# Slot 0 of a mixture-of-experts stage loaded under a count-dependent wait, and zero rows written in eight later pieces

## The chip, the cores and the metric

One core of a Trainium2 chip runs the whole kernel. The metric is the device time of one execution in microseconds; lower is better. The engines are PE (TensorE, matrix products), DVE (VectorE), ACT (ScalarE), POOL (GpSimd) and SP (SyncE, which here only issues DMAs). Each runs its own stream of instructions in program order, and semaphores hold the streams together.

## What is computed

Two attention steps, then a mixture of experts, then a dense block, all in 32-bit floats. Cut from the reference:

```python
# attention: batch 8, heads 8, seq 576, head_dim 64, 32 packs
p_packed = sm_attn(p, k, v)                  # softmax(scale * p k^T) v
out = sm_attn(q, p_packed, p_packed)
# x: 4608 tokens (batch, seq) of 512
logits = x @ w_gate                          # 8 experts
expert_idx = np.argmax(logits, axis=1)
gate_w = probs[np.arange(N), expert_idx]
for e in range(8):
    xe = x[expert_idx == e]
    h = np.maximum(xe @ w1[e], 0.0)          # 512 -> 1024
    out[mask] = gate_w[mask, None] * (h @ w2[e])   # 1024 -> 512
# dense block on the result
r = np.maximum(x @ w_in, 0.0)                # 512 -> 2048
y = (s * (r * r) + b) @ w_out                # 2048 -> 512
```

## The kernel before

**Attention stage.** 16 units of one batch and four heads each; a unit is one iteration of every engine's loop (`for it in range(UNITS ...)`), and a batch is two units. SP loads k, q and v of unit u+2 into double buffers as PE lets go of them, and in every second unit one 512 KB chunk of expert 0's weights. In an iteration PE turns k and q, makes the scores, mixes values and packs; ACT takes the exponentials and the copies out of PSUM; DVE takes maxima and sums, writes the finished rows of x into `x_rows`, and every second iteration works out each token's expert (`experts`) and its rank in that expert's list (`positions`), with PE's `ranks(b)` between them. `base` (`counts_so_far`) holds the count of tokens of each expert up to the batch last ranked.

**Rows by expert.** `rows_dram` has one region of 4608 + 128 rows for each expert. POOL's `scatter(b, j)` sends 96 rows of x, gate and token number, by an indirect DMA, to their places there; a batch has six, and counts 96 on `x_sent[b % 4]`. So that a slot of 128 rows that is not full reads zeros, the first 128 rows of every region are zeroed first: ACT issues one DMA for all eight regions before its first iteration, and POOL waits for it (`zeroed`) before the first scatter.

**Expert stage.** The lists are cut into slots of 128 tokens, an expert's slots one after the other, and an expert without tokens gets one slot. DVE works out small tables after the last ranks (`step(...)`, `tables`): for each slot the row to load (`x_at`), the row to write (`y_at`), the count of weight chunks it needs (`w_need`) and the weight buffer (`w_off`). For each slot s:

- ACT loads x (`load(s)`) into the one buffer `xin`; PE turns it (`slot_in`); ACT copies it out as the high part (`x_hi`), DVE subtracts to get the low part (`x_lo`).
- PE makes h = x w1 in 24 products (`slot_up`), ACT the relu, PE turns h (`slot_turn`), ACT and DVE split it (`h_hi`, `h_lo`), PE makes y = h w2 in 24 products (`slot_down`), ACT scales by the gate and writes y (`y_out_`).

PE's loop runs `slot_up(s)`, `slot_in(s+1)`, `slot_down(s-1)`, `slot_turn(s)`.

**Weights.** An expert has eight chunks (four of w1, four of w2), numbered on through all experts; n is the running number, `EARLY` is 8. SP may fetch chunk n when `conv` (chunks converted) is at n-1, into `raw[n % 2]`. A conversion makes a high part and a low part and then counts `conv`. Chunks 0 to 7 (expert 0) are converted in the attention stage; chunks 8 and 9 by ACT (`round_high`) and DVE (`round_low`), since their place in the second weight buffer is `x_rows`, which is free only when the scatters have landed; chunks 10 and up by POOL (`split`), which waits for all scatters and for `conv` 10 first. POOL may convert expert e's chunks when the expert before the last has made its last product:

```python
def release(o):
    done = pool.value_load(starts[0:1, bass.ds(o - 1, 1)], min_val=1, max_val=SLOTS)
    pool.wait_ge(y_full, done)
```

`release(2)` stands ahead of expert 2's chunks and waits for the last slot of expert 0, `release(3)` for that of expert 1.

**Dense stage.** Groups of 512 tokens on PE, with no part in the change.

What sets the order around the change is the order of the calls in each engine's block: ACT's `load(0)` waits for `tables` and for all of `x_sent`; behind it stand `round_high(8)`, `round_high(9)`, `x_hi(0)`. DVE ends `positions(7)`, makes the tables, then `round_low(8)`, `round_low(9)`, `x_lo(0)`, `x_lo(1)`, `h_lo(0)`.

## Time and profile before

| | |
|---|---|
| median of 3 runs | 1540.14 us (1539.99 to 1545.33) |
| the profiled execution | 1553.64 us, span 1551.9 us |
| PE busy | 1458.8 us, 94% of the span |
| DVE, ACT, POOL busy | 31%, 31%, 27% |
| chain that ended last | PE 90%, DVE 3%, issue 3%, DMA 1%, POOL 1% |
| DMA | 122.93 MB, mean 79 GB/s |

The span is the profiled execution from its first to its last instruction; the time beside it also holds what lies around the span. All times of the trace are counted from the span's start. In the span cut into 40 slices, PE's busy share and the granted clock (in tenths) are:

```profile
PE   6887369999999999998999999999999999999996
...
PEclk9899679999999999999999999999999999999998
```

The first five slices are the attention stage and the boundary behind it, the next thirteen the experts, the rest the dense stage. A slice is 38.8 us.

### The profile page before, as it was taken

Reading aid. Unit: us, or ns where it says so; the run is one execution under the profiler, and the core shown is the slowest. Engines: PE = TensorE matmul, PEld = TensorE weight load, DVE = VectorE, ACT = ScalarE, POOL = GpSimd, SP = SyncE. Lnnn points to the kernel's source line nnn. Section 1 sums busy time; section 2 is a strip of 40 time slices with the busy share of each in tenths; the row PEclk is TensorE's granted clock in tenths of the full one; section 3 lists DMA queues with packets and bytes.
Section 4 is the critical chain, followed back from the end, with each engine's and each line's share of the span. In section 5 each row is a group of like instructions: output and inputs, shape, how many; then the busy total and the mean of one; then the engine's idle time right before and its main releaser. Section 6 shows DMA issues by size and latency. Waiting matters only on the chain.

```text
span 1551.9 us, 24717 instructions
## 1 busy us (share of the span) xinstructions
PE 1458.8 (94%) x8664; PEld 1174.5 (76%) x8665; DVE 474.2 (31%) x808; ACT 480.3 (31%) x973; POOL 415.6 (27%) x278
## 2 busy tenths in 40 slices
PE   6887369999999999998999999999999999999996
PEld 5655258888888888886888888888888888888885
DVE  3777621111111111113523232322323232332322
ACT  5666123333333333332222222222222222222221
POOL 0244678448266557104501010100101010010100
PEclk9899679999999999999999999999999999999998
DMA  9688345234243343212101010100101000000000
GB/s 309 220 264 250 120 147 159 87 108 133 70 141 108 109 122 115 81 48 90 61 14 42 7 41 14 38 10 14 41 8 41 14 34 14 14 27 0 27 1 27
DMA packets 52860, 122.93 MB, mean 79 GB/s; under 512 B 6609, under 2 KB 12753, under 8 KB 52817
## 3 DMA queue, kind: packets, MB, share of 16 engines
q1 hardware_dynamic: 33728, 79.21, 16.8%
q10 hardware_dynamic: 13136, 24.19, 5.1%
q0 software_dynamic: 5952, 18.92, 3.4%
q8 instruction: 31, 0.51, 0.1%
q14 instruction: 13, 0.10, 0.0%
HBM read 90.78 MB, written 31.52 MB: 79 GB/s over the span
## 4 chain that ended last, share of the span: by engine, by line
PE 90%; DVE 3%; issue 3%; DMA 1%; POOL 1%; ACT 1%; another core or an unknown queue 0%; SPq 0%; ACTq 0%; DVEq 0%; POOLq 0%
PE psum L674 18%; PE psum L676 18%; PE psum L675 18%; PE psum L750 8%; PE psum L748 8%; PE psum L749 8%; PE psum L718 2%; PE psum L507 1%; PE psum L683 1%; PE psum L736 1%; PE psum L568 1%; PE psum L547 1%; POOL x_by_expert L418 1%; PE psum L609 1%; PE psum L622 1%
## 5 line engine op out<-in xcount | busy, mean ns | idle before, releaser
L1241 DVE SCALAR_TENSOR_TENSOR s_r_r<-r_relu,s_col 128x512 f32<-128x512 f32 x144 | 116.1, 806 | 450.4 <-ACT r_relu L972 450.4
L482 POOL DMA_INDIRECT out_dram<-out_sb,out_row_of_y x36 | 36.0, 1001 | 747.2 <-ACT out_sb L982 739.0
L674 PE MATMUL psum<-weights_split,gT_hi 128*128 128x512 f32 x576 | 230.8, 401 | 2.3 <-DVE gT_lo L1243 2.2
L972 ACT ACTIVATE r_relu<-psum 128x512 f32<-128x512 f32 x144 | 86.1, 598 | 471.7 <-PE psum L750 456.9
L675 PE MATMUL psum<-weights_split,gT_hi 128*128 128x512 f32 x576 | 227.7, 395 | 0.0
L676 PE MATMUL psum<-weights_split,gT_lo 128*128 128x512 f32 x576 | 227.6, 395 | 0.0
L750 PE MATMUL psum<-yT_hi,weights_split 128*128 128x512 f32 x576 | 227.2, 394 | 0.0
L748 PE MATMUL psum<-yT_hi,weights_split 128*128 128x512 f32 x576 | 226.1, 393 | 0.1
L749 PE MATMUL psum<-yT_lo,weights_split 128*128 128x512 f32 x576 | 225.8, 392 | 0.0
L396 POOL TENSOR_TENSOR weights_split<-weights_raw,one 128x1024 fp32r<-128x1024 f32 x70 | 135.5, 1936 | 253.9 <-PE psum L676 242.7
L398 POOL TENSOR_TENSOR weights_split<-weights_raw,weights_split 128x1024 fp32r<-128x1024 f32 x70 | 170.0, 2428 | 5.5
L1243 DVE SCALAR_TENSOR_TENSOR gT_lo<-s_r_r,b_col,gT_hi 128x512 fp32r<-128x512 f32 x144 | 114.4, 794 | 114.1 <-ACT gT_hi L975 113.3
L975 ACT ACTIVATE gT_hi<-s_r_r,b_col 128x512 fp32r<-128x512 f32 x144 | 104.3, 724 | 126.9 <-DVE s_r_r L1241 121.1
L674 PE MATMUL psum<-weights_split,hT_hi 128*128 x320 | 130.6, 408 | 4.7 <-issue 4.7
L674 PE MATMUL psum<-weights_split,xT_hi 128*128 x320 | 130.9, 409 | 2.8 <-DVE xT_lo L1217 2.8
L1223 DVE TENSOR_TENSOR hT_lo<-psum,hT_hi 128x512 fp32r<-128x512 f32 x80 | 51.5, 686 | 265.9 <-ACT hT_hi L908 265.9
L674 PEld LDWEIGHTS psum<-weights_split,gT_hi 128*128 128x128 f32 x576 | 108.3, 188 | 28.0 <-issue 2.4
L676 PEld LDWEIGHTS psum<-weights_split,gT_lo 128*128 128x128 f32 x576 | 108.2, 188 | 26.2
L749 PEld LDWEIGHTS psum<-yT_lo,weights_split 128*128 128x128 f32 x576 | 108.4, 188 | 25.8
L676 PE MATMUL psum<-weights_split,xT_lo 128*128 x320 | 127.6, 399 | 0.0
L675 PE MATMUL psum<-weights_split,xT_hi 128*128 x320 | 127.4, 398 | 0.0
L675 PE MATMUL psum<-weights_split,hT_hi 128*128 x320 | 127.2, 398 | 0.0
(151 smaller groups left out, 1832.4 us busy)
## 6 DMA issues: line engine op xcount, KB each, us to landing
weights_raw<-in_moe_w_dram SPq DMA_DIRECT2D x64, 512.0 KB
x_slot<-x_by_expert ACTq DMA_DIRECT2D x40, 257.0 KB, 2.8
y_sorted<-y_slot ACTq DMA_DIRECT2D x40, 256.5 KB, 3.3
k_sb<-in_k_dram SPq DMA_DIRECT2D x16, 576.0 KB, 6.5
q_sb<-in_q_dram SPq DMA_DIRECT2D x16, 576.0 KB, 7.7
v_sb<-in_v_dram SPq DMA_DIRECT2D x48, 192.0 KB
y_tile<-y_sorted SPq DMA_DIRECT2D x32, 256.5 KB, 2.7
weights_raw<-in_moe_w_in_dram SPq DMA_DIRECT2D x8, 512.0 KB
```

Of the source, the lines that this page charges most:

```text
L396: nc.gpsimd.tensor_tensor(hi, raw[c_ % 2][:], one[:].to_broadcast([P, CH]), ALU.mult).then_inc(hi_done, 1)
L398: nc.gpsimd.tensor_tensor(lo, raw[c_ % 2][:], hi, ALU.subtract).then_inc(conv, 1)
L674: nc.tensor.matmul(dst, lhs[0][:, col:col + P], rhs[0], start=first_, stop=False)
L675: nc.tensor.matmul(dst, lhs[0][:, col:col + P], rhs[1], start=False, stop=False)
L676: return nc.tensor.matmul(dst, lhs[1][:, col:col + P], rhs[0], start=False, stop=last_)
L748: nc.tensor.matmul(ps[:, HFB + f % 2, :], w[0], yT[0][:, k_, :], start=(k_ == 0), stop=False)
L749: nc.tensor.matmul(ps[:, HFB + f % 2, :], w[0], yT[1][:, k_, :], start=False, stop=False)
L750: last = nc.tensor.matmul(ps[:, HFB + f % 2, :], w[1], yT[0][:, k_, :], start=False, stop=(k_ == KD - 1))
L972: nc.scalar.activation(rel[:], ps[:, HFB + par, :], ACT.Relu).then_inc(rel_done, 1)
L975: nc.scalar.activation(gT[par][0][:], sq[par][:], ACT.Identity, bias=b_col[:]).then_inc(ghi_done, 1)
L1241: nc.vector.scalar_tensor_tensor(sq[par][:], rel[:], s_col[:], rel[:], ALU.mult, ALU.mult).then_inc(sq_done, 1)
L1243: nc.vector.scalar_tensor_tensor(gT[par][1][:], sq[par][:], b_col[:], gT[par][0][:], ALU.add, ALU.subtract).then_inc(glo_done, 1)
```

## The change

**Zero rows.** The one DMA of ACT becomes eight of 128 rows, issued in iterations 4 (three), 5 (three) and 6 (two), ahead of `out_pkt`. POOL waits for all eight, and sends batch 0's six scatters together after batch 2's logits.

**Slot 0's load.** It moves from ACT to SP, with a fixed address (the start of expert 0's region), behind chunk 8 and ahead of chunk 9. It no longer waits for the tables. What it waits for depends on `sent_need`, which DVE works out in iteration 15 from expert 0's count in batches 0 to 5: from 256 tokens up, only batches 0 to 5 must have landed (slots 0 and 1 are then complete), below that all eight. ACT's `load(1)` waits in the same way and for the tables.

**Order of slot 0's work.** PE takes slot 0 with fixed weights and without the tables right after `ranks(7)`: in, up, turn, then slot 1's in, slot 0's down; after it waits for the tables. ACT and DVE follow; the conversions of chunks 8 and 9 are placed anew.

```diff
@@ sync
             for n in (EARLY - 1, EARLY):
                 chunk(n % NCH, n, expert_chunk(n // NCH, n % NCH))
 
+            sp.wait_ge(need_done, 1)
+            sent = sp.value_load(sent_need[0:1, 0:1], min_val=BATCH_DMA, max_val=2 * BATCH_DMA)
+            for b in range(XBUFS):
+                sp.wait_ge(x_sent[b], 2 * BATCH_DMA if b < 2 else sent)
+            sp.wait_ge(t0_full, UNITS)
+            sp.wait_ge(t1_full, UNITS)
+            sp.dma_start(xin[:], rows_dram[0:P, :]).then_inc(xin_in, 16)
             for n in range(EARLY + 1, 2 * NCH):
                 chunk(n % NCH, n, expert_chunk(n // NCH, n % NCH))
@@ gpsimd
-                if b >= 2:
+                if b >= 3:
...
                 if b == 1:
-                    pool.wait_ge(zeroed, 16)
-                if b + 1 < B:
+                    round_low(2)
+                if b == 2:
+                    pool.wait_ge(zeroed, 16 * E)
+                    for j in range(J):
+                        scatter(0, j)
+                if 2 <= b and b + 1 < B:
                     scatter(b - 1, 0)
@@ tensor
             ranks(B - 1)
             pe.wait_ge(xa_done, UNITS)
-            pe.wait_ge(rank_read, B + 1)
-            pe.wait_ge(tables, 1)
...
             def slot_up(s):
-                ready = pe.value_load(w_need[0:1, bass.ds(s, 1)], min_val=KD, max_val=E * NCH)
-                buf = pe.value_load(w_off[0:1, bass.ds(s, 1)], min_val=0, max_val=WBUF)
+                ready, buf = KD, 0
+                if not isinstance(s, int) or s > 0:
+                    ready = pe.value_load(w_need[0:1, bass.ds(s, 1)], min_val=KD, max_val=E * NCH)
+                    buf = pe.value_load(w_off[0:1, bass.ds(s, 1)], min_val=0, max_val=WBUF)
...
-            before3 = pe.value_load(slots_m3[0:1, 0:1], min_val=N // P - 3, max_val=SLOTS - 3)
             slot_in(0)
             slot_up(0)
+            pe.wait_ge(rank_read, B + 1)
+            slot_turn(0)
             slot_in(1)
-            slot_turn(0)
-            with pe.Fori(1, before3 + 2) as s:
+            slot_down(0)
+            pe.wait_ge(tables, 1)
+            before3 = pe.value_load(slots_m3[0:1, 0:1], min_val=N // P - 3, max_val=SLOTS - 3)
+            slot_up(1)
+            slot_in(2)
+            slot_turn(1)
+            with pe.Fori(2, before3 + 2) as s:
@@ scalar
-            act.wait_ge(zeros_done, 1)
-            act.dma_start(rows_dram.rearrange("(e r) c -> r e c", e=E)[0:P],
-                          zeros[:].unsqueeze(1).to_broadcast([P, E, XW])).then_inc(zeroed, 16)
             for it in range(UNITS + 1):
...
+                if it == 4:
+                    act.wait_ge(zeros_done, 1)
+                if 4 <= it < 7:
+                    for e in range(3 * it - 12, min(3 * it - 9, E)):
+                        act.dma_start(rows_dram[e * REG:e * REG + P, :], zeros[:]).then_inc(zeroed, 16)
                 if it >= 1:
                     out_pkt(it - 1)
...
-            act.wait_ge(tables, 1)
-            before3 = act.value_load(slots_m3[0:1, 0:1], min_val=N // P - 3, max_val=SLOTS - 3)
-
-            for sent in x_sent:
-                act.wait_ge(sent, BATCH_DMA * B // XBUFS)
-            load(0)
+            act.wait_ge(x_sent[0], 2 * BATCH_DMA)
             round_high(EARLY)
             round_high(EARLY + 1)
             x_hi(0)
             keep_columns(0, 0)
+            act.wait_ge(need_done, 1)
+            sent = act.value_load(sent_need[0:1, 0:1], min_val=BATCH_DMA, max_val=2 * BATCH_DMA)
+            for b in range(XBUFS):
+                act.wait_ge(x_sent[b], 2 * BATCH_DMA if b < 2 else sent)
+            act.wait_ge(tables, 1)
+            before3 = act.value_load(slots_m3[0:1, 0:1], min_val=N // P - 3, max_val=SLOTS - 3)
             load(1)
             relu(0)
+            h_hi(0)
             x_hi(1)
             keep_columns(1, 1)
+            for sent in x_sent:
+                act.wait_ge(sent, 2 * BATCH_DMA)
             load(2)
-            h_hi(0)
@@ vector
+                if it == UNITS - 1:
+                    dve.wait_ge(rank_read, B - 1)
+                    nc.vector.tensor_scalar(few_first[:], base[0:1, 0:1], float(2 * P), float(BATCH_DMA), ALU.is_lt, ALU.mult).then_inc(few_done, 1)
...
+                if it == UNITS - 1:
+                    dve.wait_ge(few_done, 1)
+                    nc.vector.tensor_scalar_add(sent_need[:], few_first[:], float(BATCH_DMA)).then_inc(need_done, 1)
...
             positions(B - 1)
+            x_lo(0)
...
             nc.vector.tensor_tensor(y_at[:], x_f[:], x3[:, 2, :], ALU.subtract).then_inc(tables, 1)
+            dve.wait_ge(tables, 1)
+            before3 = dve.value_load(slots_m3[0:1, 0:1], min_val=N // P - 3, max_val=SLOTS - 3)
+            h_lo(0)
+            x_lo(1)
+            for sent in x_sent:
+                dve.wait_ge(sent, 2 * BATCH_DMA)
             round_low(EARLY)
             round_low(EARLY + 1)
-            dve.wait_ge(tables, 1)
-            before3 = dve.value_load(slots_m3[0:1, 0:1], min_val=N // P - 3, max_val=SLOTS - 3)
-            x_lo(0)
-            x_lo(1)
-            h_lo(0)
             with dve.Fori(1, before3 + 2) as s:
```

`slot_down` gets the same two lines as `slot_up`. The line numbers of the changed kernel differ from those of the kernel before.

**The order of instructions on DVE**, from the end of the slot tables to the slot loop, before (`slot_y_row` is the last of the tables, `weights_split` the conversions of chunks 8 and 9):

```order
L1204 CAST slot_row<-x_f 1x43 [waits rt]
L1205 TENSOR_TENSOR slot_y_row<-x_f,x 1x43
L1211 TENSOR_TENSOR weights_split<-weights_raw,weights_split 128x1024 [waits conv,hi_done] x2
L1226 TENSOR_LOAD slots_minus [waits tables]
L1226 ISA x2
L1217 TENSOR_TENSOR xT_lo<-psum,xT_hi 128x512 [waits xhi_done] x2
L1223 TENSOR_TENSOR hT_lo<-psum,hT_hi 128x512 [waits hhi_done] x2
```

In the changed kernel, first at the end of the last batch's ranks (`nslot` is the first of the tables), then from the tables' end on:

```order
L1105 TENSOR_TENSOR row_of_token_sb<-rank_of_token,region_of_token 96x6 [waits rank_sum]
L1200 TENSOR_TENSOR xT_lo<-psum,xT_hi 128x512 [waits xhi_done]
L1222 MEMSET nslot 1x2x8 x2
L1224 TENSOR_SCALAR cnt_i<-counts_so_far 1x8 [waits rank_read]
L1225 TENSOR_SCALAR cnt_i<-cnt_i 1x8 [waits rt]
```

```order
L1254 CAST slot_row<-x_f 1x43 [waits rt]
L1255 TENSOR_TENSOR slot_y_row<-x_f,x 1x43
L1258 TENSOR_LOAD slots_minus [waits tables]
L1258 ISA x2
L1206 TENSOR_TENSOR hT_lo<-psum,hT_hi 128x512 [waits hhi_done] x2
L1200 TENSOR_TENSOR xT_lo<-psum,xT_hi 128x512 [waits xhi_done]
L1196 TENSOR_TENSOR weights_split<-weights_raw,weights_split 128x1024 [waits x_sent3,hi_done,x_sent2,conv,x_sent1,x_sent0]
L1196 TENSOR_TENSOR weights_split<-weights_raw,weights_split 128x1024 [waits conv,hi_done]
```

Slot 0's `xT_lo` has moved ahead of the tables, and both conversions have moved behind slot 0's `hT_lo` and slot 1's `xT_lo`.

**On SP**, from the last v load to the chunks of expert 1, before:

```order
L318 DMA v_sb<-in_v_dram 32x4x384 [waits pk_full]
L318 DMA v_sb<-in_v_dram 32x4x384 x2
L297 DMA weights_raw<-in_moe_w_dram 128x2x512 [waits conv]
L297 DMA weights_raw<-in_moe_w_dram 128x1024 [waits conv] x4
L297 DMA weights_raw<-in_moe_w_dram 128x2x512 [waits conv] x4
```

and in the changed kernel:

```order
L321 DMA v_sb<-in_v_dram 32x4x384 [waits pk_full]
L321 DMA v_sb<-in_v_dram 32x4x384 x2
L300 DMA weights_raw<-in_moe_w_dram 128x2x512 [waits conv]
L300 DMA weights_raw<-in_moe_w_dram 128x1024 [waits conv]
L342 TENSOR_LOAD sent_before_slot [waits need_done]
L342 ISA x2
L347 DMA x_slot<-x_by_expert 128x514 [waits x_sent3,t0_full,x_sent2,t1_full,x_sent1,x_sent0]
L300 DMA weights_raw<-in_moe_w_dram 128x1024 [waits conv] x3
```

Of expert 1's four w1 chunks the first (chunk 8) still stands ahead; the other three are now behind slot 0's load and its waits.

**On ACT**, from the last exponentials to slot 0's and slot 1's loads, before:

```order
L849 ACTIVATE logits_exp<-logits_shifted 96x48 [waits exp_in] x2
L929 TENSOR_LOAD slots_minus [waits tables]
L929 ISA x2
L893 TENSOR_LOAD slot_row [waits x_sent2,x_sent3,x_sent1,x_sent0]
L893 ISA x2
L894 ISA
L894 DMA x_slot<-x_by_expert 128x514
L845 CAST weights_split<-weights_raw 128x1024 [waits raw_in0]
L845 CAST weights_split<-weights_raw 128x1024 [waits raw_in1]
L898 CAST xT_hi<-psum 128x512 [waits tx_full]
```

and in the changed kernel:

```order
L867 CAST weights_split<-weights_raw 128x1024 [waits raw_in0,x_sent0]
L867 CAST weights_split<-weights_raw 128x1024 [waits raw_in1]
L922 CAST xT_hi<-psum 128x512 [waits tx_full]
L949 COPY gate_and_token<-x_slot 128x2
L958 TENSOR_LOAD sent_before_slot [waits need_done,gid_done]
L958 ISA x2
L962 TENSOR_LOAD slots_minus [waits x_sent3,x_sent2,tables,x_sent1,x_sent0]
L962 ISA x2
L917 TENSOR_LOAD slot_row
L917 ISA x2
L918 ISA
L918 DMA x_slot<-x_by_expert 128x514
```

Slot 0's load is gone from here; the casts of chunks 8 and 9 no longer stand behind the tables and all the scatters, but still ahead of slot 0's `xT_hi`; slot 1's load now waits for the tables.

## Rows read from the trace of the kernel before

**Rows 1.** windows of the stage boundary; us, each engine's busy us (instructions), PEclk, DMA share, GB/s
```profile
180.00:200.00 20.00, 1.02 (x9) 0.97 (x9) 10.85 (x48) 0.24 (x1) 12.75 (x17) 0.50 0.44 131
```

**Rows 2.** the chain that ended last, around slot 0's load; start us, us, what
```profile
196.35 3.58 DMA x_by_expert<-x_rows,row_of_token_sb
...
200.74 2.77 DMA x_slot<-x_by_expert
```

**Rows 3.** timeline, DVE; start us, us, engine line op out<-in xcount [idle before <-releaser]
```profile
189.63 0.14 DVE L1174 TENSOR_SCALAR cnt_i<-counts_so_far 1x8 int32<-1x8 f32 x1
...
195.95 0.18 DVE L1205 TENSOR_TENSOR slot_y_row<-x_f,x 1x43 int32<-1x43 f32 x1
...
202.24 2.56 DVE L1211 TENSOR_TENSOR weights_split<-weights_raw,weights_split 128x1024 fp32r<-128x1024 f32 x2 [6.10 <-ACT weights_split L845]
...
205.32 0.69 DVE L1217 TENSOR_TENSOR xT_lo<-psum,xT_hi 128x512 fp32r<-128x512 f32 x1 [0.53 <-ACT xT_hi L898]
```

**Rows 4.** timeline, ACT, from the first conversions of expert 1 to slot 0's relu
```profile
201.16 1.99 ACT L845 CAST weights_split<-weights_raw 128x1024 fp32r<-128x1024 f32 x2 [13.88 <-issue]
...
204.70 0.59 ACT L898 CAST xT_hi<-psum 128x512 fp32r<-128x512 f32 x1 [1.55 <-PE psum L683]
...
206.08 0.35 ACTq L894 DMA_DIRECT2D x_slot<-x_by_expert  x1
...
214.72 0.60 ACT L903 ACTIVATE h_relu<-psum 128x512 f32<-128x512 f32 x1 [2.34 <-PE psum L676]
```

**Rows 5.** timeline, POOL, conversions of expert 1's last six chunks and after
```profile
207.12 1.89 POOL L396 TENSOR_TENSOR weights_split<-weights_raw,one 128x1024 fp32r<-128x1024 f32 x1 [9.85 <-DMA weights_raw<-in_moe_w_dram]
...
213.39 2.37 POOL L398 TENSOR_TENSOR weights_split<-weights_raw,weights_split 128x1024 fp32r<-128x1024 f32 x1
...
230.93 2.41 POOL L398 TENSOR_TENSOR weights_split<-weights_raw,weights_split 128x1024 fp32r<-128x1024 f32 x1
...
233.30 1.90 POOL L396 TENSOR_TENSOR weights_split<-weights_raw,one 128x1024 fp32r<-128x1024 f32 x1
...
291.94 1.90 POOL L396 TENSOR_TENSOR weights_split<-weights_raw,one 128x1024 fp32r<-128x1024 f32 x1 [23.81 <-PE psum L676]
```

**Rows 6.** timeline, PE, products of slots 0 to 2
```profile
206.26 0.79 PE L674 MATMUL psum<-weights_split,xT_hi 128*128 x1 [1.59 <-DVE xT_lo L1217]
...
214.95 1.07 PE L718 MATMUL psum<-ident,h_relu 128*128 128x128 f32 x8
...
229.80 0.48 PE L674 MATMUL psum<-weights_split,xT_hi 128*128 x1
...
235.83 0.48 PE L674 MATMUL psum<-weights_split,hT_hi 128*128 x1
```

**Rows 7.** timeline, SP's queue, chunk 10 (two issues)
```profile
203.49 1.66 SPq L297 DMA_DIRECT2D weights_raw<-in_moe_w_dram  x2
```

**Rows 8.** the line of the zero rows' DMA (L861)
```profile
DMA to landing us min/median/max: 19.0/19.0/19.0
```

**Rows 9.** timeline, PE, attention stage, units 2 to 5 (L547 opens an iteration)
```profile
27.17 0.71 PE L547 MATMUL psum<-kqT,pT_of_unit 64*32 64x288 f32 x16
...
31.04 1.51 PE L507 MATMUL psum<-ident,k_sb 128*128 128x128 f32 x6 [2.25 <-DMA k_sb<-in_k_dram]
...
38.54 0.72 PE L547 MATMUL psum<-kqT,pT_of_unit 64*32 64x288 f32 x16 [0.18 <-issue]
...
46.03 0.72 PE L547 MATMUL psum<-kqT,pT_of_unit 64*32 64x288 f32 x16
...
57.14 1.21 PE L547 MATMUL psum<-kqT,pT_of_unit 64*32 64x288 f32 x16
```

**Rows 10.** timeline, POOL, scatters of batches 0, 1 and 7
```profile
88.57 0.19 POOL L416 COPY x_rows<-token_of_row 96x6 f32<-96x6 f32 x1
...
105.81 0.92 POOL L418 DMA_INDIRECT x_by_expert<-x_rows,row_of_token_sb  x1 [3.83 <-DVE a L1102]
...
196.35 0.92 POOL L418 DMA_INDIRECT x_by_expert<-x_rows,row_of_token_sb  x1 [0.30 <-issue]
```

35 lines of the change are left out of this document (20 added, 15 removed).

## The prediction

> **What bounds the kernel now.** I read the windows first, then the chain of waits, then the timelines of POOL, DVE, ACT, PE and SP around 175 to 292 us, and last the start of the attention stage. From 217 us to the end PE is almost always busy, so nothing is to be had there except a new gap. The hole is between the stages: from 180 to 200 us PE works 1.02 us of 20, at the lower granted clock [rows 1]. The chain shows what fills it: POOL's scatters, the landing of the last one 3.58 us after its issue at 196.35, and slot 0's x rows, issued at 200.74 and landed 2.77 us later [rows 2]. Then come `x_hi`, `x_lo` and the first product at 206.26 [rows 3, 4, 6]. The change wants slot 0's products before the last scatters have landed.
>
> **Which way the new wait goes.** The threshold is 256 tokens of expert 0 in batches 0 to 5; below it SP waits for every scatter, as ACT did. The trace says which it is. POOL converts expert 2's weights into slot 0's buffer only after `release(2)`, that is after the last product of expert 0. It starts them at 233.30, right behind expert 1's, with no wait [rows 5]. PE starts slot 1's down products only at 235.83 [rows 6], so at 233.30 only slot 0 was complete: expert 0 has one slot, at most 128 tokens. (The next release comes at 291.94, after slot 5 [rows 5].) So the new condition takes its long branch, and slot 0 is not loaded earlier. What is left is the new order.
>
> **Slot 0 in the new order, on the clock of the trace of before.**
> 1. SP's address is constant and its register is read long before, so the load goes out when the last scatter has landed (196.35 + 3.58 = 199.9) and not 0.8 later [rows 2]: 200.05, landed 202.8.
> 2. SP's chunk 9 now stands behind that load; before it was fetched while the scatters ran. Issued at 200.5, it takes what chunk 10 takes, issued 203.49 and there at 207.12 [rows 5, 7], 3.6 us, plus 0.2 for sharing: 204.3. ACT's cast of chunk 9 (1.0 each [rows 4]) stands before `x_hi(0)`: 205.3, then 0.6 for `x_hi` and 0.75 with the handover for `x_lo` [rows 3, 4]: 206.65. PE starts slot 0 at 206.9, **0.65 later** than 206.26.
> 3. `x_lo(0)` now stands ahead of the slot tables on DVE. They took 189.63 to 196.13 [rows 3], 6.5 us under the scatters; now 206.65 to 213.15. ACT's load of slot 1 waits for them, with some 0.9 of register reads: issue 214.1, landed 216.9. ACT's `relu(0)` is behind it but is hardly late, since its second half needs the end of slot 0's up products: 8.46 us after their start (206.26 to 214.72 [rows 4, 6]), 215.35.
> 4. DVE's `round_low(8)` and `round_low(9)`, run at 202.24 before, now stand behind `h_lo(0)` and `x_lo(1)`, that is behind slot 0's up products. `relu` ends at 215.95, the turn of h at 216.6, slot 1's x is turned at 217.5, `x_hi(1)` ends at 218.1, `x_lo(1)` at 218.85 (each by the duration of its like [rows 3, 4, 6]). So `round_low(8)` runs from 218.9, **16.7 later**.
> 5. SP's chunk 10 waits for it, and POOL's first conversion for the chunk: 207.12 becomes 223.8. The six conversions left of expert 1 take 207.12 to 233.34 [rows 5], 26.2 us, with nothing to shorten them: done at 250.0.
> 6. PE: slot 0's down products run from 218.2 to 223.8, earlier in order than before, then PE waits for chunk 11 (223.8 + 8.6 = 232.4). Slot 1's up products follow, the lower clock's 8.5 us, 2.1 us of relu and split, slot 2's up products 5.7 (229.80 on, before 235.83 [rows 6]): about 249. The same set of work is then done as before at 235.83, when slot 1's down products begin. They need all of expert 1's chunks: 250.0, so **+14.2**; 2.5 us of the 16.7 are the slack between 233.34 and 235.83 [rows 5, 6]. From there PE never stood still for weights before (POOL stood idle from 268 to 291.94 [rows 5]), so nothing gives the 14.2 back.
>
> The edits of steps 2 to 5 are not on the trace together; I bound their sum by 11 (loads landing at once, no sharing) and 17 (each handover 0.3 dearer). I take 14.2, the sum of the rows.
>
> **Zero rows.** One DMA of 2.1 MB took 19.0 us to land [rows 8], in the time of the first k, q and v loads. PE waited 2.25 us for unit 3's k at 31.04, and that iteration lasted 27.17 to 38.54 = 11.4 us, the next 38.54 to 46.03 = 7.5 [rows 9]. **Gain: up to 3.9 us.** Eight pieces later give some back: ACT issues three, three and two inside an iteration, about 0.4 each as ACT's issues take [rows 4], 3 us in all, of which ACT's short idle stretches there hide about half; and the same bytes pass beside the loads of units 6 to 8. **Back: 1.4.** Net -2.5, between -7.6 and +3. The Trainium skill says (DMA: Bandwidth & Descriptors, "Issuing engines are not separate DMA queues") that DMAs from ACT, SP and GpSimd run on the same 16 engines and interleave; the 19.0 us and the late k agree. By that rule the bytes only move, and the gain holds only so far as the new place is less full; were the queues independent, this term would be -0 and +1.4.
>
> POOL's move of batch 0's scatters costs nothing: six in a row and two of batch 1 end near 99, and the wait that follows, for DVE, ended at 105.81 after 3.83 us of idleness [rows 10]. That idle time is the cover; without it the burst would cost about 3 us. The two instructions on DVE for `sent_need`: 0.3 us, beside waits.
>
> **Sum.** 14.2 - 2.5 = +11.7. The profiled execution (1553.64, span 1551.9) would take 1565.3. The median of the runs, 1540.14, is 13.5 below it; I put the difference on the median: **1551.8 us**, 0.8% slower. Half a per cent, 7.7 us, is about what a measurement of this kernel can tell from none.
>
> **Rivals.**
> - *The start of attention gains more.* Iteration 4 also lasted 11.1 us (46.03 to 57.14) against 7.5 [rows 9], with a stop and a low clock after it. Were that gone too, the stage gains 3.9 + 3.6 = 7.5: 1540.1 + 14.2 - 7.5 = 1546.8, **no measurable change**. For it: that stop comes in full DMA traffic. Against: the new pieces go out just there. Chance 0.12.
> - *Slot 0 does start early, on the other side.* Place: SP's wait for batches 0 to 5. From 256 tokens up the twelve scatters of batches 6 and 7, 1.22 us each [rows 10], are no longer ahead of slot 0: -14.6, and with -2.5 about 1523, **faster**. It needs expert 0 to own at least two slots; rows 5 say one. Chance 0.02. A change that does not do what it says is my forecast itself.
> - *The stage gives back more.* The ACT issues cost their full 3 us and the loads wait for the pieces: the attention term is +1 to +3, time 1556. Chance 0.13.
> - *Zeros late.* Batch 0's scatters wait for all eight pieces. The last two go out near 67; if each took the 19.0 us of the whole [rows 8], they land at 86, and the scatters come at 88.57 [rows 10]. Only beyond that would it cost, some 3 us: 1555. The skill (same page, "Rules for kernel authors") says to coalesce small transfers into large ones, and that page counts about 2 us of fixed cost for each DMA. By it eight pieces carry an estimated 14 us more of fixed cost; no run here shows whether in series. Chance 0.03.
>
> The forecast keeps 0.70. Slower by over 0.5%: 0.70 + 0.13 + 0.03 = 0.86, less 0.01 for its low tail, 0.85; within 0.5%: 0.13; faster: 0.02. The range: 11 - 5 = +6 at the low end (1546) and 17 + 1.5 = +18.5 at the high end (1558.6); it takes in the first, third and fourth rivals and leaves out the tails and the early start.
>
> **What would show it.** In the profile after: the x load on SP near 200, the tables (DVE) after the first `xT_lo` and not before 196; both `round_low` on DVE after `hT_lo`; POOL's first conversion of chunk 10 some 17 us later than 207; a gap of about 8 us in PE before slot 1's up products, with the lower clock behind it; slot 1's down products some 14 us late; everything after at the old pace. The k wait at 31 gone. I am wrong if SP's load goes out before the last scatter, if POOL starts before 215, or if PE shows no gap after slot 0's down products.

## The result, and the profile after

| | before | after |
|---|---|---|
| median of the runs, us | 1541.79 (1539.99 to 1545.33, 4 runs) | 1565.36 (1562.68 to 1569.08, 4 runs) |
| profiled execution, us | 1553.64, span 1551.9 | 1569.08, span 1567.3 |

The ratio is 1.0146, 95% interval [1.0126, 1.0166]: 22.5 us slower (the two medians of four runs differ by 23.6). The direction of the forecast held; its size, 11.7 us, was half of what came, and the time lies outside the range.

The boundary between the stages first. In the changed kernel L428 is the scatter, L1200 `x_lo`, L1206 `h_lo`, L1196 DVE's `round_low`, L406 and L408 POOL's two halves of a conversion, and L686 a product. SP's queue:

```profile
196.53 0.34 SPq L347 DMA_DIRECT2D x_slot<-x_by_expert  x1
196.92 41.25 SPq L300 DMA_DIRECT2D weights_raw<-in_moe_w_dram  x7
```

POOL's timeline from the last scatter on:

```profile
193.01 0.92 POOL L428 DMA_INDIRECT x_by_expert<-x_rows,row_of_token_sb  x1 [0.31 <-issue]
220.59 1.89 POOL L406 TENSOR_TENSOR weights_split<-weights_raw,one 128x1024 fp32r<-128x1024 f32 x1 [26.66 <-DMA weights_raw<-in_moe_w_dram]
246.87 1.89 POOL L406 TENSOR_TENSOR weights_split<-weights_raw,one 128x1024 fp32r<-128x1024 f32 x1 [0.45 <-DMA weights_raw<-in_moe_w_dram]
```

DVE's, with what it waited for:

```profile
201.98 0.69 DVE L1200 TENSOR_TENSOR xT_lo<-psum,xT_hi 128x512 fp32r<-128x512 f32 x1 [15.63 <-ACT xT_hi L922]
212.75 1.29 DVE L1206 TENSOR_TENSOR hT_lo<-psum,hT_hi 128x512 fp32r<-128x512 f32 x2 [3.78 <-ACT hT_hi L932]
214.34 0.69 DVE L1200 TENSOR_TENSOR xT_lo<-psum,xT_hi 128x512 fp32r<-128x512 f32 x1 [0.30 <-ACT xT_hi L922]
```

and PE's:

```profile
202.82 0.77 PE L686 MATMUL psum<-weights_split,xT_hi 128*128 128x512 f32 x1 [2.42 <-DVE xT_lo L1200]
214.13 0.47 PE L686 MATMUL psum<-weights_split,hT_hi 128*128 128x512 f32 x1 [0.45 <-issue]
229.30 0.79 PE L686 MATMUL psum<-weights_split,xT_hi 128*128 x1 [9.36 <-POOL weights_split L408]
246.78 0.49 PE L686 MATMUL psum<-weights_split,hT_hi 128*128 x1 [0.24 <-issue]
```

SP's load of slot 0 goes out 3.5 us behind the last scatter: it waited for all of them. POOL, which stood 9.85 us idle ahead of chunk 10 before [rows 5], now stands 26.66. PE waits 9.36 us for POOL ahead of slot 1's up products, and slot 1's down products (the last PE row) begin 53.77 us behind the last scatter; in the profile of before it was 235.83 - 196.35 = 39.48 [rows 2, 6].

The attention stage, PE's timeline (L561 opens an iteration; these are units 2 to 5) and ACT's issues of the zero rows:

```profile
30.05 0.72 PE L561 MATMUL psum<-kqT,pT_of_unit 64*32 64x288 f32 x16
37.51 0.72 PE L561 MATMUL psum<-kqT,pT_of_unit 64*32 64x288 f32 x16
44.99 0.72 PE L561 MATMUL psum<-kqT,pT_of_unit 64*32 64x288 f32 x16
48.30 0.25 PE L572 MATMUL psum<-wg_sb,pkT 64*32 64x8 f32 x8 [2.33 <-ACT pkT L847]
57.32 0.24 PE L636 MATMUL psum<-v_sb,a1T 96*32 96x64 f32 x1 [3.81 <-issue]
58.96 1.21 PE L561 MATMUL psum<-kqT,pT_of_unit 64*32 64x288 f32 x16
```
```profile
45.10 2.79 ACTq L891 DMA_DIRECT2D x_by_expert<-zeros  x3
```

The wait for unit 3's k is gone, and unit 2's iteration takes 7.5 us instead of 11.4 [rows 9]. But unit 4's takes 14.0 instead of 11.1: ACT is busy for 2.79 us with three issues, `pkT` comes late by 2.33, and a stop of 3.81 follows.

### The profile page after: what moved, and what is told of

Read it like the earlier page. It is cut to its first block, busy times and chain, and to the rows that moved or that the text cites. A ratio compares the mean times of both kernels' runs of the same rounds, so it can differ in the third digit from the quotient of the medians.

```text
span 1567.3 us, 24677 instructions
## 1 busy us (share of the span) xinstructions
PE 1467.9 (94%) x8664; PEld 1177.8 (75%) x8665; DVE 475.8 (30%) x810; ACT 480.1 (31%) x973; POOL 416.5 (27%) x278
## 4 chain that ended last, share of the span: by engine, by line
PE 88%; DVE 3%; issue 3%; DMA 2%; POOL 2%; ACT 1%; ACTq 0%; SPq 0%; DVEq 0%; POOLq 0%
PE psum L686 18%; PE psum L688 18%; PE psum L687 18%; PE psum L772 8%; PE psum L771 8%; PE psum L770 8%; PE psum L734 2%; PE psum L521 2%; PE psum L695 1%; PE psum L758 1%; DMA q_sb<-in_q_dram 1%; POOL x_by_expert L428 1%; PE psum L623 1%; PE psum L561 1%; PE psum L636 1%
## 5 line engine op out<-in xcount | busy, mean ns | idle before, releaser
L496 POOL DMA_INDIRECT out_dram<-out_sb,out_row_of_y x36 | 36.3, 1008 | 750.0 <-ACT out_sb L1009 741.8
L686 PE MATMUL psum<-weights_split,gT_hi 128*128 128x512 f32 x576 | 230.2, 400 | 2.2 <-DVE gT_lo L1278 2.2
L406 POOL TENSOR_TENSOR weights_split<-weights_raw,one 128x1024 fp32r<-128x1024 f32 x70 | 135.3, 1933 | 270.0 <-PE psum L688 242.0
L408 POOL TENSOR_TENSOR weights_split<-weights_raw,weights_split 128x1024 fp32r<-128x1024 f32 x70 | 169.7, 2425 | 5.5
L686 PE MATMUL psum<-weights_split,xT_hi 128*128 (+1 forms) x320 | 131.8, 412 | 13.0 <-POOL weights_split L408 9.4
L686 PE MATMUL psum<-weights_split,hT_hi 128*128 (+1 forms) x320 | 130.8, 409 | 5.5 <-issue 5.5
L1206 DVE TENSOR_TENSOR hT_lo<-psum,hT_hi 128x512 fp32r<-128x512 f32 x80 | 51.5, 686 | 266.6 <-ACT hT_hi L932 266.6
L686 PEld LDWEIGHTS psum<-weights_split,gT_hi 128*128 128x128 f32 x576 | 108.2, 188 | 29.0 <-issue 3.8
L688 PE MATMUL psum<-weights_split,xT_lo 128*128 (+1 forms) x320 | 128.2, 401 | 0.0
L688 PE MATMUL psum<-weights_split,hT_lo 128*128 (+1 forms) x320 | 128.0, 400 | 0.0
L687 PE MATMUL psum<-weights_split,xT_hi 128*128 (+1 forms) x320 | 128.0, 400 | 0.0
L770 PEld LDWEIGHTS psum<-yT_hi,weights_split 128*128 128x128 f32 x576 | 108.3, 188 | 26.0
```

The lines of the kernel that those rows point to most:

```text
L406: nc.gpsimd.tensor_tensor(hi, raw[c_ % 2][:], one[:].to_broadcast([P, CH]), ALU.mult).then_inc(hi_done, 1)
L408: nc.gpsimd.tensor_tensor(lo, raw[c_ % 2][:], hi, ALU.subtract).then_inc(conv, 1)
L686: nc.tensor.matmul(dst, lhs[0][:, col:col + P], rhs[0], start=first_, stop=False)
L687: nc.tensor.matmul(dst, lhs[0][:, col:col + P], rhs[1], start=False, stop=False)
L688: return nc.tensor.matmul(dst, lhs[1][:, col:col + P], rhs[0], start=False, stop=last_)
L770: nc.tensor.matmul(ps[:, HFB + f % 2, :], w[0], yT[0][:, k_, :], start=(k_ == 0), stop=False)
```

## The experiments

Each kernel ran beside the kernel before on one chip; a ratio is to those runs. The timed sets fell on five chips, whose own medians of the kernel before were 1545.69, 1546.34, 1556.67, 1542.65 and 1544.57. "Boundary" is the time from the last scatter's issue to slot 1's first down product, "rest" from there to the last instruction on POOL. In the profile of before the rest is 1306.07 us, in the changed kernel's 1310.61: 4.5 more, in stages in which the change touches nothing.

### The change in two parts

**c_again** is the kernel before, unchanged.

> The kernel before, unchanged, profiled once more. Theory 1 (the profiled execution of before was a slow draw in the attention stage: it took 1553.6 us against a median of 1541.8): here the last scatter is issued 5 to 10 us before 196.35 and the stage from there to slot 1's down products is as long as it was (39.5 us). Theory 2 (the profiled one was ordinary and the 12 us lie elsewhere): the last scatter again near 196. Time within 3 us of the kernel before.

1545.41 us, ratio 1.0004 [0.9988, 1.0019]. Boundary 38.73, rest 1305.74. Its last scatter is issued here:

```profile
188.59 0.92 POOL L418 DMA_INDIRECT x_by_expert<-x_rows,row_of_token_sb  x1 [0.30 <-issue]
```

That is 7.8 us sooner than in the profile that I predicted from [rows 2], so that execution was slow in its attention stage. I compare from here on with c_again.

**zeros_only** is the kernel before with the zero rows and their scatters alone as in the change; **slot_only** is the changed kernel with the zeros and the scatters as before.

> Only the zero rows' part of the change (eight pieces in iterations 4 to 6, batch 0's scatters together). Theory 1 (this part costs the attention stage time, which the slow draw of before hid): +9 us, about 1551, with the last scatter later than in the kernel before profiled beside it. Theory 2 (as predicted, it gains): -2.5 us, about 1539. Rival (it does nothing, and the slot part costs all of the 23.6 us): within 2 us of before.

> Only slot 0's part of the change, with the zero rows in one early DMA and batch 0's scatters as before. Theory 1: +14 us, about 1556 (the 14.3 us that the profile shows between the last scatter and slot 1's down products). Rival (the slot part costs all): +23 us, 1565. In both POOL's first conversion of chunk 10 stands 27.5 us behind the last scatter, against 10.8 before.

zeros_only: 1549.68 us, ratio 1.0031 [1.0011, 1.005], **+4.8 us**; boundary 38.77, rest 1306.03, so in its profile only the attention stage differs. slot_only: 1566.67, ratio 1.0138 [1.011, 1.0167], **+21.3**; boundary 53.87, rest 1310.94. So the slot part has two terms: 15.1 at the boundary and 5 behind it.

### The boundary

**conv_ahead**, the changed kernel with DVE's conversions ahead of `h_lo(0)` and `x_lo(1)`, but still behind `x_lo(0)` and the tables:

```diff
+            for sent in x_sent:
+                dve.wait_ge(sent, 2 * BATCH_DMA)
+            round_low(EARLY)
+            round_low(EARLY + 1)
             dve.wait_ge(tables, 1)
...
             h_lo(0)
             x_lo(1)
-            for sent in x_sent:
-                dve.wait_ge(sent, 2 * BATCH_DMA)
-            round_low(EARLY)
-            round_low(EARLY + 1)
```

> The changed kernel with DVE's conversions of chunks 8 and 9 (and their wait for all scatters) ahead of h_lo(0) and x_lo(1), still behind the slot tables. Theory (the order on DVE sets POOL's chain): POOL starts chunk 10 some 7 us earlier after the last scatter (20.5 instead of 27.5), the gap of 9.4 us in PE shrinks to 3 or less, time 7 us under the changed kernel, about 1558. Rival (chunk 9 behind slot 0's load sets it): no more than 1 us under the changed kernel.

1563.38 us, ratio 1.0121 [1.0096, 1.0145]. POOL's chunk 10 starts 21.04 us behind the last scatter instead of 27.58, and the boundary is 48.33: 5.4 us of 15 are back there. (One slot later, at slot 2's down products, it is 4.0, since slot 1's waited 3.64 us for POOL; the ratios, 1.0146 and 1.0121, differ by 3.9 us.) The tables still stand ahead of the conversions; the next kernel moves them as well.

**dve_old** is the changed kernel with DVE's whole order of before:

```diff
-            x_lo(0)
...
+            for sent in x_sent:
+                dve.wait_ge(sent, 2 * BATCH_DMA)
+            round_low(EARLY)
+            round_low(EARLY + 1)
             dve.wait_ge(tables, 1)
...
-            h_lo(0)
-            x_lo(1)
+            x_lo(0)
+            x_lo(1)
+            h_lo(0)
```

> The changed kernel with VectorE in the order of the kernel before: tables, the wait for all scatters, the two conversions, then x_lo(0), x_lo(1), h_lo(0). Theory (the boundary's 15 us are VectorE's two conversions that stand behind h_lo(0) and x_lo(1), so that GpSimd's conversion of expert 1 starts late): GpSimd's first conversion of chunk 10 starts 11 us behind the last scatter and slot 1's down products 39 to 40 us behind it, as in the kernel before; the median is 14 us under the changed kernel, 1551. Rival (the conversions ahead gave back 5.4 us of 15 already, and what is left comes from ScalarE, whose conversions now stand behind other work, or from chunk 9's raw weights behind slot 0's load): slot 1's down products still over 43 us behind the last scatter, 1555 to 1560. The 1310 us behind it stay as they are by either.

1553.26 us, ratio 1.0057 [1.0035, 1.008]. POOL's timeline, and PE's:

```profile
186.27 0.92 POOL L428 DMA_INDIRECT x_by_expert<-x_rows,row_of_token_sb  x1 [0.30 <-issue]
196.90 1.89 POOL L406 TENSOR_TENSOR weights_split<-weights_raw,one 128x1024 fp32r<-128x1024 f32 x1 [9.70 <-DVE weights_split L1196]
```
```profile
197.38 0.76 PE L686 MATMUL psum<-weights_split,xT_hi 128*128 128x512 f32 x1 [3.32 <-DVE xT_lo L1200]
209.04 0.47 PE L686 MATMUL psum<-weights_split,hT_hi 128*128 128x512 f32 x1 [2.69 <-issue]
```

POOL starts 10.63 us behind the last scatter, as in the kernel before (c_again 10.68), and the boundary is 42.85. So 10.9 of the 15 us are DVE's order. The 4.1 left stand in PE's two rows: slot 0's up products wait 3.32 for `xT_lo` (1.59 before [rows 6]), since chunk 9's cast now waits for a load behind slot 0's; and slot 0's down products, now with no up products of slot 1 ahead of them to cover the split of h, come 2.69 late. The first belongs to SP's order and the second to PE's; I did not part them further.

**early**: the wait that the change was built for, forced. With this input the reference sends no token at all to expert 0, so its rows are zeros whichever scatters have landed.

```diff
-...base[0:1, 0:1], float(2 * P), float(BATCH_DMA), ALU.is_lt, ALU.mult)...
+...base[0:1, 0:1], float(-1), float(BATCH_DMA), ALU.is_lt, ALU.mult)...
```

> The changed kernel with the other branch of its wait taken always: the compare of expert 0's count is made with -1 instead of 256, so that sent is 96 and slot 0's load waits for the scatters of batches 0 to 5 only. With this input expert 0 has no tokens, so its rows are the zeros either way. Theory: slot 0's products then follow the last ranks and lie beside the last batches' scatters, but GpSimd's conversions of expert 1 still wait for all scatters, and GpSimd has 14 chunks' work behind them, which still sets when slot 1's up products can run: slot 1's down products come 5 to 15 us sooner after the last scatter than in the changed kernel (39 to 49 us instead of 53.8), median 1550 to 1560. Rival, the price in my prediction for slot 0 early (1523): all of slot 0's up and down products come off the path, 25 to 30 us behind the last scatter, median 1535 or less.

1553.57 us, ratio 1.0059 [1.0036, 1.0082]; boundary 39.19. PE's timeline (the last scatter goes out at 188.83):

```profile
183.81 0.77 PE L686 MATMUL psum<-weights_split,xT_hi 128*128 128x512 f32 x1 [1.49 <-DVE xT_lo L1200]
195.61 0.47 PE L686 MATMUL psum<-weights_split,hT_hi 128*128 128x512 f32 x1 [0.29 <-issue]
210.54 0.79 PE L686 MATMUL psum<-weights_split,xT_hi 128*128 x1 [9.11 <-POOL weights_split L408]
```

Slot 0 is indeed done by 201, and it buys nothing against the kernel before: slot 1 waits 9.11 us for POOL's conversion of expert 1, which starts at 201.83. The early start that I priced at 1523 us is refuted for this code.

**early_conv**: `early` with DVE's conversions sooner. The low half of chunk 8 overwrites x rows of batches 2 and 6 only.

```diff
             x_lo(0)
+            dve.wait_ge(x_sent[2], 2 * BATCH_DMA)
+            round_low(EARLY)
...
+            for sent in x_sent:
+                dve.wait_ge(sent, 2 * BATCH_DMA)
+            round_low(EARLY + 1)
             dve.wait_ge(tables, 1)
...
-            for sent in x_sent:
-                dve.wait_ge(sent, 2 * BATCH_DMA)
-            round_low(EARLY)
-            round_low(EARLY + 1)
```

> The kernel 'early' (slot 0 loaded behind batches 0 to 5) with VectorE's two conversions moved: chunk 8's low half right behind x_lo(0), under a wait for the scatters of batches 2 and 6 alone, whose buffer it writes over; chunk 9's ahead of h_lo(0), behind all scatters. Theory (with slot 0 out of the way the boundary is GpSimd's conversion of expert 1 alone, and its start hangs on these two): GpSimd's first conversion of chunk 10 starts 5 to 7 us behind the last scatter instead of 13.0, and slot 1's down products come 31 to 34 us behind it instead of 39.2; the median is 6 us under 'early', 1547 or less. Rival (raw weights or x_slot come late behind the scatters whatever GpSimd does): over 37 us.

1562.63 us, ratio 1.0037 [1.0019, 1.0055] (on the slow chip). POOL's chunk 10 starts 6.15 us behind the last scatter and the boundary is **32.40**, as forecast. The median moved less than forecast: 3.4 us under `early` by the ratios instead of 6. With slot 0 out of the way GpSimd's conversion sets the boundary, and its start hangs on two DVE subtractions.

**conv_sooner** is the kernel before with the same two conversions sooner, and ACT's casts of chunks 8 and 9 ahead of its waits for the tables and the scatters.

```diff
+            act.wait_ge(x_sent[0], 2 * BATCH_DMA)
+            round_high(EARLY)
+            round_high(EARLY + 1)
             act.wait_ge(tables, 1)
...
             load(0)
-            round_high(EARLY)
-            round_high(EARLY + 1)
```

> The kernel before with the same two conversions sooner: ScalarE rounds chunks 8 and 9 behind the scatters of batches 0 and 4 only, ahead of the tables, VectorE makes chunk 8's low half right behind the last ranks and chunk 9's behind all scatters. Theory (in the kernel before the boundary is slot 0's own chain of load, turn, up and down products, and GpSimd has slack): GpSimd's chunk 10 starts 5 to 7 us behind the last scatter instead of 10.7, but slot 1's down products only 1 to 1.5 us sooner (37 to 38 us behind it), since ScalarE's casts of 2 us no longer stand ahead of xT_hi; the median within 2 us of the kernel before. Rival (GpSimd sets the boundary there too): slot 1's down products 4 to 5 us sooner, the median 1541 to 1542.

1557.38 us, ratio 1.0003 [0.9988, 1.0017]; POOL starts 5.48 us behind the last scatter instead of 10.68, and the boundary is still 38.73: not even the forecast 1 us. In the kernel before slot 0's own chain binds, and POOL has slack.

### Behind the boundary

Each tile of the dense stage takes 22.68 us in c_again and 22.77 in all kernels with the new slot order above: 0.09 us on each of 36 tiles, 3.2 us. I first took TensorE's longer program for the cause.

**peeled** is the kernel before with the first round of TensorE's slot loop written out:

```diff
-            with pe.Fori(1, before3 + 2) as s:
+            slot_up(1)
+            slot_in(2)
+            slot_down(0)
+            slot_turn(1)
+            with pe.Fori(2, before3 + 2) as s:
```

> The kernel before with one edit: the first iteration of TensorE's slot loop is written out (slot_up(1), slot_in(2), slot_down(0), slot_turn(1), then the loop from 2), so that TensorE's program gets as long as in the changed kernel, with the order of the work untouched. Theory L (the 5 us that all three kernels with the new slot order lose after slot 1's down products come from TensorE's longer code, which puts the dense loop elsewhere): from slot 1's down products to the last instruction 1310 to 1311 us instead of 1305.7 to 1306.1, and the median 4 to 5 us over the kernel before. Rival S (they come from the order of the work at the boundary, by the buffers and the transfers that it sets going): 1306 us and no difference in the median, within 0.15%.

1544.09 us, ratio 0.9989 [0.997, 1.0009]; rest 1305.58, and 26 of its 30 tiles take 22.68. A miss for my theory.

**after_pad** and **before_pad** add 45 and 120 semaphore increments to TensorE's program, in the kernels after and before:

```diff
+            for _ in range(45):
+                pe.sem_inc(pads, 1)
             ranks(B - 1)
             pe.wait_ge(xa_done, UNITS)
```

> The changed kernel with 45 increments of a semaphore that nobody waits for on TensorE, ahead of the wait for the last x, where TensorE stands idle anyway. They bring TensorE's program to the length of 'peeled', which ran the stages behind the boundary in 1305.6 us. Theory P (the 4.6 us behind the boundary hang on where TensorE's dense loop lies in the program): 1305.5 to 1307 us from slot 1's down products to the last instruction, every dense tile 22.68 us instead of 22.77, and the median 4 us under the changed kernel. Rival S (they come from the state in which the new order leaves the engines, whatever the code's place): 1310 to 1311 us and 22.77 us a tile, no change in the median.

> The kernel before with 120 such increments at the same place: the 60 matmuls with their 60 weight loads that the changed kernel has more on TensorE ahead of the dense loop. TensorE stands idle for some 14 us there, so the increments cost the boundary nothing to 1 us. Theory P: 1310 us from slot 1's down products to the end, 22.77 us a tile, the median 4 to 5 us over the kernel before. Rival S: 1305.7 us, 22.68 us a tile, no change in the median.

after_pad: 1584.78 us, ratio 1.0173 [1.0149, 1.0197]; before_pad: 1567.08, ratio 1.0052 [1.0032, 1.0072]. Both are slower than expected, by my fault: the increments stand ahead of the last ranks, and not behind, and in both kernels the last ranks, on which the last scatters wait, come later. The dense tiles answer the question all the same: still 22.77 in after_pad, still 22.68 in before_pad. The place of the code is not it. (The rests are 1308.17 and 1307.42.)

What was left is where the data lies. The change's two small tensors are allocated in the middle of SBUF, and each takes 32 bytes, so every tensor behind them moves up by 64, the dense stage's among them (`gT_hi0` from 169920 to 169984).

**before_shift** is the kernel before with these two tensors, unused, and no other difference:

```diff
+        sb("expert_0_is_short", [1, 1])
+        sb("sent_before_slot_1", [1, 1], I32)
         starts = sb("slot_starts", [1, E + 1], I32)
```

> The kernel before with one edit: the two small tensors that the change adds on SBUF (expert_0_is_short, sent_before_slot_1) are allocated at the change's place and never used. As in the changed kernel every tensor behind them lies 64 bytes higher, the dense stage's gT, yT, r_relu, s_r_r and out_sb among them. No instruction differs. Theory A (the 3 to 5 us behind the boundary come from these addresses): every dense tile 22.77 us instead of 22.68, the dense stage 713 us instead of 710, and the median 3 to 4 us over the kernel before. Rival S (they come from the order or the program, not the addresses): 22.68 us and no difference in the median.

PE's timeline at the start of four tiles, c_again's:

```profile
906.84 0.60 PE L736 MATMUL psum<-ident,y_tile 128*128 128x128 f32 x4
929.53 0.60 PE L736 MATMUL psum<-ident,y_tile 128*128 128x128 f32 x4
952.21 0.60 PE L736 MATMUL psum<-ident,y_tile 128*128 128x128 f32 x4
974.89 0.60 PE L736 MATMUL psum<-ident,y_tile 128*128 128x128 f32 x4
```

and before_shift's:

```profile
904.10 0.60 PE L738 MATMUL psum<-ident,y_tile 128*128 128x128 f32 x4
926.88 0.60 PE L738 MATMUL psum<-ident,y_tile 128*128 128x128 f32 x4
949.65 0.60 PE L738 MATMUL psum<-ident,y_tile 128*128 128x128 f32 x4
972.42 0.60 PE L738 MATMUL psum<-ident,y_tile 128*128 128x128 f32 x4
```

Three tiles take 68.05 us in the one and 68.32 in the other, with no instruction changed. The windows of the two show TensorE busy all the time at clock 1.00 in both (884 and 880 matmul records in 200 us):

```profile
800.00:1000.00 200.00, 200.00 (x884) 162.49 (x883) 61.80 (x86) 54.68 (x96) 11.92 (x12) 1.00 0.09 28
```
```profile
800.00:1000.00 200.00, 200.00 (x880) 161.74 (x879) 61.63 (x85) 54.15 (x94) 12.02 (x12) 1.00 0.08 28
```

The last stretch, from the last y tile to the end, which holds the last four tiles' products, takes 104.1 us against 103.5 or 103.6 in kernels with the tensors in the old place; with the 32 tiles before it that would make some 3.4 us. Against c_again's trace, in which four tiles take 22.77 as well, the tiles and the last stretch are 2.7 us longer, and the whole rest, 1308.08, is 2.3 longer. The changed kernel's tiles and last stretch are 3.4 us longer than c_again's.

That leaves 1.4 of the changed kernel's 4.9 us. They stand in the hand-over to the dense stage, from the first `y_tile` to the fourth: 58.78 us against 57.41. The first 32 us of it in c_again, in the changed kernel and in `together` (below); the granted clock is the third number from the end:

```profile
690.60:722.60 32.00, 24.89 (x110) 19.80 (x111) 9.63 (x9) 7.64 (x18) 10.55 (x5) 0.95 0.23 75
```
```profile
710.20:742.20 32.00, 25.20 (x105) 20.02 (x106) 9.11 (x9) 6.96 (x16) 9.36 (x5) 0.89 0.21 71
```
```profile
686.70:718.70 32.00, 25.32 (x102) 20.02 (x103) 9.27 (x9) 6.84 (x16) 9.48 (x5) 0.86 0.20 69
```

TensorE's clock has two levels, 2.4 and 1.2 GHz. In these stretches, with the same four stops of TensorE, c_again spends one spell of 3.4 us at the lower level, the changed kernel two and `together` three. pieces_only, burst_only and before_pad, with the old slot order, have two as well; early and dve_old, with the new one, have one. So one profile of each does not show that the change causes the second spell.

before_shift's median, 1544.96, ratio 1.0009 [0.9993, 1.0025], is 1.4 us up, with an interval that holds 0 as well as these 3.4.

**after_noshift** is the changed kernel with the two tensors at byte 228864, above all others.

```diff
-        few_first = sb("expert_0_is_short", [1, 1])
-        sent_need = sb("sent_before_slot_1", [1, 1], I32)
...
+        c = ExitStack()
+        sb("below_few", [P, 16272], scope=c)
+        few_first = sb("expert_0_is_short", [1, 1], scope=c)
+        sent_need = sb("sent_before_slot_1", [1, 1], I32, scope=c)
+        c.close()
```

> The changed kernel with the two small tensors at the top of SBUF (byte 228864), so that every other tensor lies where it does in the kernel before. Theory A: dense tiles of 22.68 us, 1306 to 1307.5 us behind slot 1's down products, the median 3 to 4.5 us under the changed kernel, at 1.011 to 1.012 of the kernel before. Rival S: 22.77 us, 1310 us, and 1.0146 as the changed kernel.

1561.3 us, ratio 1.0124 [1.0098, 1.015] against 1.0146; nearly all tiles take 22.68, and the last stretch 103.5. The rest is 1308.32, so 2.6 us over c_again's are still there. 1.5 of them are a second spell at the lower clock in the hand-over (58.93 us), some 0.5 stand in the expert slots, and 0.5 in three tiles that carry a stop of 0.25 to 0.5 us, where c_again has one. Single profiles of kernels with the old slot order spread as far (1308.80 in pieces_only, 1307.18 in burst_only).

### The zero rows

**pieces_only** has ACT's eight pieces and the scatters' old order, **burst_only** the one transfer and the scatters' new order:

```diff
+                if it == 4:
+                    act.wait_ge(zeros_done, 1)
+                if 4 <= it < 7:
+                    for e in range(3 * it - 12, min(3 * it - 9, E)):
+                        act.dma_start(rows_dram[e * REG:e * REG + P, :], zeros[:]).then_inc(zeroed, 16)
```
```diff
-                if b >= 2:
+                if b >= 3:
...
                 if b == 1:
-                    pool.wait_ge(zeroed, 16)
-                if b + 1 < B:
+                    round_low(2)
+                if b == 2:
+                    pool.wait_ge(zeroed, 16)
+                    for j in range(J):
+                        scatter(0, j)
+                if 2 <= b and b + 1 < B:
```

> The kernel before with ScalarE's eight pieces of zeros in iterations 4 to 6 and GpSimd's scatters in their old order. Theory Q (most of zeros_only's loss is at the pieces: ScalarE's issues of 2 to 4 us, the late pkT, the stops behind them): iterations 4 and 5 take 24 us together instead of 20, the k wait of iteration 2 is gone, and the median is 1 to 3 us over the kernel before. Rival R (the loss is the burst of six scatters): the median 3 us under the kernel before, as I predicted for the k wait.

> The kernel before with its one transfer of zeros and the changed order of batch 0's scatters: none in batch 1's time, six in a row in batch 2's, and the third conversion moved. Theory Q: one iteration near 90 us gets 2 to 4 us longer and a later one shorter, and the median is 0 to 2 us over the kernel before. Rival R: 4 to 7 us over it.

pieces_only: 1547.51 us, ratio 1.0031 [1.0019, 1.0043], +4.8 us. burst_only: 1543.80, ratio 1.001 [0.9996, 1.0024], between 0.6 us under and 3.7 over the kernel before. So the pieces alone cost as much as both parts did; the burst's own part is not clear of nothing, though in its profile the iteration at 91 us takes 12.7 us, 8.4 in before_shift. PE's timeline in pieces_only, units 2 to 5:

```profile
27.43 0.72 PE L547 MATMUL psum<-kqT,pT_of_unit 64*32 64x288 f32 x16
34.88 0.72 PE L547 MATMUL psum<-kqT,pT_of_unit 64*32 64x288 f32 x16
42.36 0.72 PE L547 MATMUL psum<-kqT,pT_of_unit 64*32 64x288 f32 x16
45.49 0.24 PE L558 MATMUL psum<-wg_sb,pkT 64*32 64x8 f32 x8 [2.15 <-ACT pkT L825]
54.30 0.22 PE L622 MATMUL psum<-v_sb,a1T 96*32 96x64 f32 x1 [3.50 <-issue]
55.32 1.21 PE L547 MATMUL psum<-kqT,pT_of_unit 64*32 64x288 f32 x16
```

Units 2 to 5 take 7.5, 7.5, 13.0 and 11.7 us; in before_shift, on the same chip, 13.6, 8.0, 9.8 and 10.6. That is a gain of 6.6 and a loss of 4.3, so this profile ought to be 2.3 us ahead. It is: its last scatter goes out at 183.77, before_shift's at 185.70. But this one execution is a quick one (1543.3 us; the median of 12 is 1547.5), so it does not show where the median loses its 4.8 us. zeros_only's does so in part. Up to the end of unit 5 it is 0.8 us ahead of c_again: 5.5 gained in units 2 and 3, 4.7 given back in units 4 and 5. Behind that it loses 3.5 us, with long iterations in units 8 and 12 (13.1 and 12.5 us; c_again has 9.5 in unit 12 and 11.9 in unit 14); but peeled, with the old zeros and scatters, has the same two (13.1 and 12.7). Whether the new zeros make such iterations more frequent stays open.

The stop ahead of unit 4's last product (the row at 54.30) is in c_again too, with 2.14 us instead of 3.50. The packets of the traces suggest what it is: in c_again, pieces_only, zeros_only and the changed kernel it ends 1.3 to 1.4 us behind the end of a 16 KB packet of the queue that the page lists as "instruction" (in pieces_only 52.0 to 53.0 us). TensorE seems to wait for its own instructions there. No run varied that.

**zeros_spread** issues the pieces on SP, two each behind the values of units 3 to 6, with the old scatters, to spare ACT:

```diff
                 load_v(u)
+                if u == 3:
+                    sp.wait_ge(zeros_done, 1)
+                if 3 <= u < 7:
+                    for e in range(2 * u - 6, 2 * u - 4):
+                        sp.dma_start(rows_dram[e * REG:e * REG + P, :], zeros[:]).then_inc(zeroed, 16)
```

> The kernel before with the zero rows in eight pieces, but from SP's queue behind the values of units 3 to 6, two at a time, and GpSimd's scatters in their old order. Theory (the eight pieces take away the wait for k at 31 us, and what zeros_only paid was ScalarE's issues of 2.3 to 3.9 us in iteration 4 and the burst of six scatters at 85 to 100 us): iteration 2 takes 7.5 to 9.5 us instead of 13, the last scatter comes 3 us sooner than in the kernel before run beside it, and the median is 2 to 4 us under it. Rival (bandwidth: 2.1 MB cost their time wherever they stand ahead of the scatters, since the stage waits for k, q and v): the waits for k and q come back in iterations 3 to 6, the median within 1.5 us of the kernel before or over it.

1549.70 us, ratio 1.0026 [1.0008, 1.0044]: no gain. The rival was right. The wait for k has moved, from 30 us to 48.31, and grown to 4.35 (2.25 in the profile of before, 1.06 in c_again); that iteration takes 17.8 us. The Trainium skill (DMA: Bandwidth & Descriptors, "Issuing engines are not separate DMA queues") says that DMAs issued by ACT, SP and GpSimd run on the same 16 engines and interleave. This run agrees for SP. For ACT the eight pieces show no such wait: in zeros_only and pieces_only unit 5's k comes in time, and TensorE waits for `pkT` instead.

### Put together

**together** is slot_only with the wait forced as in `early`, the conversions of `early_conv` and the tensors out of the way. It reads slot 0 right only because expert 0 gets nothing in the last two batches.

> The slot part of the change alone (zeros and their scatters as before), with three edits: the wait for slot 0 taken as in 'early', VectorE's two conversions as in 'early_conv', and the two small tensors at the top of SBUF. Theory: 32.4 us from the last scatter to slot 1's down products instead of 39, dense tiles of 22.68 us, and nothing from the zeros, so the median is 5 to 7 us under the kernel before (0.9955 to 0.9968). Rival (something of the new slot order still costs behind the boundary, as early_conv's 1310 us there said): 0 to 3 us under it.

1540.86 us, ratio **0.998 [0.9966, 0.9995]**: 3.1 us under the kernel before (0.8 to 5.3), less than the forecast 5 to 7, and the only kernel of the study that is clear of it on the fast side. The boundary is 31.66, 7.1 less than c_again's. But slot 2's down products are only 5.5 nearer to the last scatter than there, since TensorE also waits for POOL ahead of slot 1's:

```profile
194.29 1.89 POOL L410 TENSOR_TENSOR weights_split<-weights_raw,one 128x1024 fp32r<-128x1024 f32 x1 [4.43 <-DVE weights_split L1194]
```
```profile
220.60 0.50 PE L686 MATMUL psum<-weights_split,hT_hi 128*128 x1 [2.74 <-POOL weights_split L412]
```

Behind them this profile gives back 5.0 more: 2.7 in the hand-over to the dense stage (60.16 us against 57.41, with the three spells at the lower clock shown above), 1.2 in the slots ahead of it and 1.0 in tiles. From the last scatter to its last instruction this execution is thus only 0.5 us ahead of c_again. It is a slow one (1544.60 us; the median of 12 is 1540.86), so where the median gains its 3.1 us is not shown.

**late_count** makes the branch hold for any input: slot 0 waits for batches 6 and 7 only where expert 0 is short and gets tokens in them.

```diff
+            nc.vector.tensor_scalar(late[:], base[0:1, 0:1], count_5[:, 0:1], few_first[:, 0:1], ALU.subtract, ALU.mult).then_inc(few_done, 1)
+            dve.wait_ge(few_done, 3)
+            nc.vector.tensor_scalar(sent_need[:], late[:], float(BATCH_DMA), float(BATCH_DMA), ALU.min, ALU.add).then_inc(need_done, 1)
```

> As 'together', but with a branch that holds for any input: slot 0 waits for batches 6 and 7 only if expert 0 has under 256 tokens by batch 5 and gets more in batches 6 and 7, which VectorE works out in two operations behind the last ranks; slot 1's load waits for all scatters. Here expert 0 gets none, so slot 0 is loaded some 1 us later than in 'together'. Theory: GpSimd's conversions still set the boundary, 32.4 to 34.5 us, and the median 3 to 7 us under the kernel before. Rival (slot 1's load, now 5 us behind the last scatter and behind relu(0), sets it): 36 us or more, and 0 to 3 us under.

1546.21 us, ratio 1.0017 [1.0002, 1.0032]: a miss. ACT's timeline:

```profile
185.22 1.04 ACT L869 CAST weights_split<-weights_raw 128x1024 fp32r<-128x1024 f32 x1 [9.66 <-DMA weights_raw<-in_moe_w_dram]
186.16 0.58 ACT L922 CAST xT_hi<-psum 128x512 fp32r<-128x512 f32 x1
```

Slot 0 is turned at 181.94, but `x_hi(0)` stands behind the cast of chunk 9, whose load stands behind slot 0's on SP. The tables and the conversions wait behind `x_lo(0)`, and POOL starts 12.67 us behind the last scatter instead of 5.35. The boundary is 39.09. POOL does not set it, though: TensorE waits for none of its conversions here, but for `x_lo(0)` and for slot 1's x, whose load stands behind `relu(0)`. The rival was right.

```profile
187.61 0.76 PE L688 MATMUL psum<-weights_split,xT_hi 128*128 128x512 f32 x1 [4.59 <-DVE xT_lo L1199]
200.18 0.66 PE L697 MATMUL psum<-ident,x_slot 128*128 128x128 f32 x4 [2.60 <-DMA x_slot<-x_by_expert]
```

## Why the prediction was right and wrong

**Which way the wait goes**: right. One slot for expert 0 (it has no tokens at all) was enough to see that SP would wait for all scatters.

**The slot part, steps 1 to 6**: right, nearly to the microsecond. In us behind the last scatter, forecast (from 196.35) and profile after (from 193.01):

| step | forecast | after |
|---|---|---|
| slot 0's load issued | 3.7 | 3.5 |
| slot 0's first product | 10.6 | 9.8 |
| slot 1's load issued | 17.8 | 17.3 |
| DVE's conversions start | 22.6 | 21.9 |
| POOL's chunk 10 | 27.5 | 27.6 |
| slot 1's up products | 36.1 | 36.3 |
| slot 1's down products | 53.7 | 53.8 |

The +14.2 became +14.3 against the profile of before and +15.0 against c_again. dve_old and conv_ahead confirm the cause, in part: 10.9 us are DVE's order (tables and products ahead of the conversions), 4.1 are PE's and SP's, which in the changed kernel lie under the longer wait and come out when it is taken away.

**"Everything after at the old pace"**: the first failed step. The rest took 4.9 us longer than in c_again. I costed the two added tensors at nothing, without naming them. 3.4 of the 4.9 us are dense tiles of 22.77 us instead of 22.68 and a longer last stretch; before_shift shows the same tiles without any other change, 2.7 us by its trace. The other 1.4 are a second spell at the lower clock in the hand-over, which kernels without the change have too. On the medians the tensors' price is not clear of nothing: before_shift's interval holds 0, and after_noshift gets back 3.4 by the ratios (1.0146 to 1.0124, on different chips, with intervals as wide).

**Zero rows, -2.5**: the second failed step. The gain at unit 3's k was there (3.9 forecast, 3.9 in the profile after). The "back: 1.4" was mis-sized: zeros_only cost +4.8 [1.7, 7.7], so by the median some 8 to 9 us are given back (with the 3.9 gained). I had ACT's issues at 0.4 us each; the first three took 2.79 together in the profile after, with a late `pkT` and a longer stop behind. These I can point to, 4.7 us over units 4 and 5 in zeros_only; the rest I cannot place. The rule that the bytes only move, which I let stand beside the sum, was nearer to what came than the sum; my rival "the stage gives back more" had the right sign and ended at +3.

**The sum**: 15.0 + 3.4 + 4.8 = 23.2 against 22.5 measured, as near as terms with intervals of 2 to 3 us each can be expected to come. The range ended at +18.5, for want of a term for what the list of edits did not seem to touch; it also took in only +1.5 of the +3 that my own rival allowed the attention stage. Putting the difference on the median was sound: the profile that I read had 7.8 us more than c_again's ahead of its last scatter and nearly the same behind it (a boundary of 39.48 and a rest of 1306.07, against 38.73 and 1305.74).

**Slot 0 early, 1523**: the mechanism did not come with this input, and its price was wrong as well. I had slot 0's early start at -14.6; forced in `early`, it leaves the boundary at 39.19 us, against 38.73 in c_again. I priced slot 0's way and forgot that slot 1's stands just behind it, in POOL's conversions.

## What to carry to other kernels

When an engine's order is changed, follow each engine that converts or loads for the *next* item, not only those that serve the moved one: here 11 us went through two subtractions of 1.3 us that had been put behind a product. An item taken off a path pays only down to the next chain, so time that one (here GpSimd's six conversions) before pricing the gain. Put new small tensors where nothing lies behind them, and if a stage whose instructions did not change gets slower, compare the tensors' addresses.

## What the runs showed of the hardware

- **64 bytes in SBUF change TensorE's pace.** With `gT`, `yT` and the others 64 bytes higher, a dense tile of about 100 matmuls takes 22.77 us instead of 22.68 at clock 1.00, in all eight kernels with the shift, against mostly 22.68 in those without, after_noshift, together and late_count with the new slot order among them. Up to eight of 30 tiles take 22.77 in unshifted kernels too (in the profile of before and in pieces_only), so the address may favour a state more than make it; which of the moved tensors matters was not tried. The Trainium skill (SBUF — State Buffer, "Operand start alignment") asks only for a multiple of the element's size, which both places meet.
- **Semaphore increments on TensorE are not free.** Without them TensorE pauses for 8.6 us ahead of the last ranks and goes on when DVE's `expert_onehot` is there. With 120 of them the pause is 17.34 us, and TensorE comes 6.5 us later than `expert_onehot`. With 45 it is 10.98 and still ends with `expert_onehot`, so these fit into the pause. As an estimate from the two rows: at most 17.34 / 120 = 145 ns each and, if both rows of increments begin alike, at least (17.34 - 10.98) / 75 = 85 ns. DVE itself came later in both (it stood 9.4 us idle ahead of its first read of the last unit's products; 5.71 in conv_sooner, on the same chip), and why is open.

```profile
200.60 0.54 PE L587 MATMUL psum<-counts_so_far,ident 96*96 96x56 f32 x2 [17.34 <-issue]
```
```profile
200.85 0.54 PE L601 MATMUL psum<-counts_so_far,ident 96*96 96x56 f32 x2 [10.98 <-DVE expert_onehot L1084]
```

- **Chips differ.** The median of the kernel before was 1556.67 us on one chip and 1542.65 to 1546.34 on four others. On the slow one the later attention iterations alternate between 10.7 and 8.7 us instead of 8.4, as they do in the profile that I predicted from.
